# Six pieces of 128 to 512 tokens instead of 192 to 512, the weight split in quarters, and new orders of the engines' queues

## The reference

```python
# attention: q, k, v are (4, 8, 576, 64)
scores = scale * np.matmul(q, k.transpose(0, 1, 3, 2))
kth = np.partition(scores, -32, axis=-1)[..., -32:-31]
scores = np.where(scores >= kth, scores, -1e9)
attn = np.exp(scores - np.max(scores, axis=-1, keepdims=True))
attn = attn / (np.sum(attn, axis=-1, keepdims=True) + 1e-09)
x = attn @ v                      # laid out as (2304, 512)
# first MLP, d_ff 1536
x = (1 / (1 + np.exp(-(x @ w_gate))) * (x @ w_val)) @ w_out
# second MLP, d_ff 2048
r = np.maximum(x @ w_in, 0); out = (r * r) @ w_out2
```

## Time and profile before

| | |
|---|---|
| runs | 1176.04, 1176.14, 1177.05 us |
| profiled execution | 1176.16 us |
| its span | 1174.3 us |
| busy: PE, PEld | 1132.5 us (96%), 998.2 (85%) |
| busy: DVE, ACT, POOL | 838.3 (71%), 676.4 (58%), 623.5 (53%) |
| DMA | 270.13 MB, mean 230 GB/s |
| mean granted TensorE clock | 0.984 |

### The profile page before, as it was taken

One profiled execution on the slowest core, in us unless ns is written; L12 is line 12 of the kernel. 1 busy time (PEld: TensorE's weight loads), 2 busy tenths in 40 slices (PEclk: granted clock), 3 DMA queues, 4 the chain that ended last, 5 costly groups with the idle time before them and its releaser, 6 DMA issues.

```text
span 1174.3 us, 21809 instructions
## 1 busy us (share of the span) xinstructions
PE 1132.5 (96%) x7520; PEld 998.2 (85%) x7520; DVE 838.3 (71%) x1756; ACT 676.4 (58%) x1758; POOL 623.5 (53%) x539
## 2 busy tenths in 40 slices
PE   4579999999999999999999999999999999999999
PEld 2459989999989999999888787888888888899998
DVE  7999998788997898999777688975666683011130
ACT  5886777776875765776565557755544464112130
POOL 4987687776885555675445436643443365012130
PEclk7789999999999999999999999999999999999999
DMA  9988877988888666767655555665455555577784
GB/s 356 349 307 286 281 264 246 311 274 290 274 281 310 217 213 222 217 226 234 207 164 174 178 177 192 211 197 187 172 165 172 172 163 172 192 250 250 257 252 139
DMA packets 90397, 270.13 MB, mean 230 GB/s; under 512 B 10032, under 2 KB 16176, under 8 KB 90288
## 3 DMA queue, kind: packets, MB, share of 16 engines
q1 hardware_dynamic: 90288, 268.74, 68.5%
HBM read 228.33 MB, written 40.37 MB: 229 GB/s over the span
## 4 chain that ended last, share of the span: by engine, by line
PE 88%; DVE 7%; issue 2%; ACT 1%; SPq 1%; POOL 1%; DMA 1%; ACTq 0%; POOLq 0%
PE ps L648 21%; PE ps L650 21%; PE ps L649 21%; PE ps L634 7%; PE ps L589 7%; PE ps L549 6%; PE ps L565 5%; DVE work L850 3%; DVE top L848 3%; DMA heads_in<-qk_in 1%; SPq L470 1%; DVE g_lo L885 1%; POOL below L917 0%; POOL full_buf L957 0%; POOL probs L922 0%
## 5 line engine op out<-in xcount | busy, mean ns | idle before, releaser
L848 DVE MAX8 top<-work 128x8 f32<-128x576 f32 x432 | 312.3, 751 | 0.5
L917 POOL TENSOR_TENSOR below<-scores,below 128x576 f32<-128x576 f32 x120 | 174.2, 1451 | 237.8 <-ACT below L700 237.6
L648 PE MATMUL ps<-xy_hi,ring 128*128 128x512 f32 (+2 forms) x800 | 286.4, 358 | 0.0
L650 PE MATMUL ps<-xy_hi,ring 128*128 128x512 f32 (+2 forms) x800 | 281.4, 352 | 0.0
L649 PE MATMUL ps<-xy_lo,ring 128*128 128x512 f32 (+2 forms) x800 | 281.1, 351 | 0.0
L850 DVE MATCH_REPLACE8 work<-top,work 128x576 f32<-128x576 f32 x288 | 214.1, 743 | 0.0
L648 PE MATMUL ps<-g_hi,ring 128*128 128x384 f32 (+2 forms) x560 | 200.4, 358 | 0.3 <-DVE g_lo L885 0.3
L650 PE MATMUL ps<-g_hi,ring 128*128 128x384 f32 (+2 forms) x560 | 196.9, 352 | 0.0
L649 PE MATMUL ps<-g_lo,ring 128*128 128x384 f32 (+2 forms) x560 | 196.8, 351 | 0.0
L648 PEld LDWEIGHTS ps<-xy_hi,ring 128*128 128x128 f32 x800 | 150.2, 188 | 18.5 <-issue 6.9
L650 PEld LDWEIGHTS ps<-xy_hi,ring 128*128 128x128 f32 x800 | 150.1, 188 | 12.9
(11 more groups left out here) (70 smaller groups left out, 1709.8 us busy)
## 6 DMA issues: line engine op xcount, KB each, us to landing
ring<-w_split SPq DMA_DIRECT2D x318, 512.0 KB, 4.2
wring<-w_in SPq DMA_DIRECT2D x113, 256.0 KB, 5.3
w_split<-stage SPq DMA_DIRECT2D x46, 512.0 KB, 4.7
w_split<-ring SPq DMA_DIRECT2D x22, 512.0 KB, 6.0
vt<-v_in SPq DMA_DIRECT2D x16, 480.0 KB, 6.0
heads_in<-qk_in SPq DMA_DIRECT2D x16, 336.0 KB, 4.6
vt<-v_in SPq DMA_DIRECT2D x16, 320.0 KB, 3.2
heads_in<-qk_in SPq DMA_DIRECT2D x16, 304.0 KB, 4.4
```

The costliest lines, as they stand in the source:

```text
L648: nc.tensor.matmul(dst, w_hi, hi[:, k, 0:WIDTH[c]], start=first, stop=False)
L650: mm = nc.tensor.matmul(dst, w_lo, hi[:, k, 0:WIDTH[c]], start=False, stop=final)
L848: nc.vector.max(out=best, in_=sc if step == 0 else wk).then_inc(sel_step[t % 2], 1)
L917: nc.gpsimd.tensor_tensor(out=below[:, t % 2, :], in0=scores_of(t), in1=below[:, t % 2, :], op=ALU.subtract).then_inc(mask_done, 1)
```

## The change

The six pieces hold 128, 256, 384, 512, 512 and 512 tokens. WHEN sets which blocks are split when: of four, one ahead of the MLPs, one with the first piece and two beside the second. Margins in MLP_AT, the slot of turns in the later pieces (now t+3 everywhere but in the first), the slots of the splits ahead (0 to 9 now), and the order within a slot on ScalarE, VectorE and GpSimd change; it differs between the slots up to MLP_AT[2] and those from there on. TensorE's loop is written twice, with the old order in both. The planner's tables after: MLP_AT 11, 29, 55, 85, 118, 150; 18, 26, 30, 33 and 32 slots beside pieces one to five; 17 splits ahead, 17 with the first piece, 34 beside the second; 119 whole loads and 306 of both parts; 36 groups. Scores by stage 12+0, 4+0, 12+4, 11+7, 14+5, 11+0; turns 4+0, 9+0, 12+1, 12+7, 12+8, 15+0; products 4+0, 8+0, 13+1, 11+7, 12+8, 16+0.

```diff
--- before.py
+++ after.py
@@ -23,7 +23,7 @@
 KFULL = NBLK // 2
 
 
-PIECES = (((0, 0, 3),), ((1, 0, 5),), ((0, 3, 6),), ((1, 5, 4), (2, 0, 4)), ((2, 4, 5), (3, 0, 3)), ((3, 3, 6),))
+PIECES = (((0, 0, 2),), ((0, 2, 4),), ((1, 0, 6),), ((0, 6, 3), (2, 0, 5)), ((1, 6, 3), (3, 0, 5)), ((2, 5, 4), (3, 5, 4)))
 NC = len(PIECES)
 
 NW = 1
@@ -95,9 +95,10 @@
 AHEAD = 4
 STORE_LAG = 2
 CLASSES = NW + 2
-JOBS = [(None, n, True, True) for n in range(0, NB, CLASSES)]
+WHEN = [(0,1,2,2)[n % 4] for n in range(NB)]
+JOBS = [(None, n, True, True) for n in range(NB) if WHEN[n] == 0]
 NPRE = len(JOBS)
-JOBS += [(c, n, c + 1 == n % CLASSES, c < NW or c == NW and n % CLASSES == CLASSES - 1)
+JOBS += [(c, n, c + 1 == WHEN[n], c < NW or c == NW and WHEN[n] == CLASSES - 1)
          for c in range(NC) for n in range(NB)]
 NWHOLE = NPRE + NW * NB
 
@@ -144,14 +145,15 @@
 
 
 MASK = 2
-MLP_AT = [CHUNK_END[c] + (4, 6, 7, 7, 7, 7)[c] for c in range(NC)]
+MLP_AT = [CHUNK_END[c] + (4, 6, 8, 6, 7, 7)[c] for c in range(NC)]
 PAIRED = 2
+LATE = 1
 NORM_AT, TURN_AT, PROD_AT = {}, {}, {}
 for _t in range(NT):
-    _late = UNITS[TILES[_t][0]][0] > 0
+    _late = UNITS[TILES[_t][0]][0] >= LATE
     NORM_AT[_t + 2 + _late] = _t
     if _t in UNIT_AT:
-        TURN_AT[_t + 2 + _late + (UNITS[TILES[_t][0]][0] >= PAIRED)] = UNIT_AT[_t]
+        TURN_AT[_t + 2 + _late] = UNIT_AT[_t]
 TURN_SLOT = {u: s for s, u in TURN_AT.items()}
 
 
@@ -276,7 +278,7 @@
 
 SPLIT_AT = {}
 for _k in range(NPRE):
-    SPLIT_AT.setdefault(1 + _k * (MLP_AT[0] - 2) // NPRE, []).append(_k)
+    SPLIT_AT.setdefault(_k * (MLP_AT[0] - 1) // NPRE, []).append(_k)
 
 
 def attention_mlps(nc, qk, v, w, w_split, out):
@@ -656,7 +658,25 @@
-            for s in range(SLOTS):
+            for s in range(MLP_AT[2]):
...
+            for s in range(MLP_AT[2], SLOTS):
...
@@ -806,30 +826,54 @@
                 if s == MLP_AT[0] - 1:
                     for u in PROD_AT[s]:
                         copy_x(u)
-            for s in range(MLP_AT[0], SLOTS):
+            for s in range(MLP_AT[0], MLP_AT[2]):
+                if s - MASK < NT:
+                    find_below(s - MASK)
+                    enlarge(s - MASK)
+                for u in SCORE_AT.get(s - 1, [])[-1:]:
+                    for t in tiles_of(u):
+                        copy_scores(t)
+                for c, n in blocks_of(SHARES[s - 1][2]):
+                    evac(c, n)
+                if s - 1 in TURN_AT:
+                    copy_pt(TURN_AT[s - 1])
+                for c, p in X_AT.get(s, []):
+                    split_x(c, p)
+                for c, n in blocks_of(SHARES[s][0]):
+                    evac(c, n)
+                if s - MASK < NT:
+                    exp(s - MASK)
+                for u in SCORE_AT.get(s, [])[:-1]:
+                    for t in tiles_of(u):
+                        copy_scores(t)
+                for c, n in blocks_of(SHARES[s][1]):
+                    evac(c, n)
+                for u in PROD_AT.get(s, []):
+                    copy_x(u)
+            for s in range(MLP_AT[2], SLOTS):
                 for u in SCORE_AT.get(s - 1, [])[-1:]:
                     for t in tiles_of(u):
                         copy_scores(t)
                 if s - MASK < NT:
                     find_below(s - MASK)
                     enlarge(s - MASK)
-                for c, n in blocks_of(SHARES[s - 1][2]):
-                    evac(c, n)
                 if s - 1 in TURN_AT:
                     copy_pt(TURN_AT[s - 1])
+                for c, n in blocks_of(SHARES[s - 1][2]):
+                    evac(c, n)
                 for c, n in blocks_of(SHARES[s][0]):
                     evac(c, n)
                 for u in SCORE_AT.get(s, [])[:-1]:
                     for t in tiles_of(u):
                         copy_scores(t)
+                if s - MASK < NT:
+                    exp(s - MASK)
                 for c, p in X_AT.get(s, []):
                     split_x(c, p)
-                if s - MASK < NT:
-                    exp(s - MASK)
-                for c, n in blocks_of(SHARES[s][1]):
-                    evac(c, n)
                 for u in PROD_AT.get(s, []):
                     copy_x(u)
+                for c, n in blocks_of(SHARES[s][1]):
+                    evac(c, n)
             for c, n in blocks_of(SHARES[SLOTS - 1][2]) + blocks_of(REST):
                 evac(c, n)
 
@@ -850,12 +894,9 @@
                     nc.vector.match_replace(out=wk, in_to_replace=best, in_values=sc if step == 1 else wk,
                                             imm_value=-3.0e38).then_inc(sel_step[t % 2], 1)
 
-            def select_both(s, steps):
-                for step in steps:
-                    if 0 <= s - 1 < NT and step < 3:
-                        select(s - 1, 4 + step)
-                    if s < NT:
-                        select(s, step)
+            def select_if(t, step):
+                if 0 <= t < NT:
+                    select(t, step)
 
             def invert(t):
                 dve.wait_ge(sum_done, t + 1)
@@ -887,21 +928,42 @@
                                             op=ALU.subtract).then_inc(sq_lo_done, 1)
 
             dve.wait_ge(const_ready, 1)
-            for s in range(SLOTS):
-                if s in NORM_AT and s >= MLP_AT[0]:
+            for s in range(MLP_AT[2]):
+                if s in NORM_AT and UNITS[TILES[NORM_AT[s]][0]][0] >= LATE:
                     invert(NORM_AT[s])
+                select_if(s - 1, 4)
                 for c, n in blocks_of(SHARES[s - 1][2]) if s else []:
                     evac(c, n)
-                select_both(s, [0])
-                select_both(s, [1])
+                select_if(s, 0)
+                select_if(s - 1, 5)
                 for c, n in blocks_of(SHARES[s][0]):
                     evac(c, n)
-                select_both(s, [2])
-                if s in NORM_AT and s < MLP_AT[0]:
+                select_if(s, 1)
+                select_if(s - 1, 6)
+                select_if(s, 2)
+                for c, n in blocks_of(SHARES[s][1]):
+                    evac(c, n)
+                select_if(s, 3)
+                if s in NORM_AT and UNITS[TILES[NORM_AT[s]][0]][0] < LATE:
                     invert(NORM_AT[s])
+            for s in range(MLP_AT[2], SLOTS):
+                select_if(s, 0)
+                if s in NORM_AT and UNITS[TILES[NORM_AT[s]][0]][0] >= LATE:
+                    invert(NORM_AT[s])
+                select_if(s, 1)
+                for c, n in blocks_of(SHARES[s - 1][2]) if s else []:
+                    evac(c, n)
+                select_if(s - 1, 4)
+                select_if(s, 2)
+                if s in NORM_AT and UNITS[TILES[NORM_AT[s]][0]][0] < LATE:
+                    invert(NORM_AT[s])
+                select_if(s - 1, 5)
+                for c, n in blocks_of(SHARES[s][0]):
+                    evac(c, n)
                 for c, n in blocks_of(SHARES[s][1]):
                     evac(c, n)
-                select_both(s, [3])
+                select_if(s - 1, 6)
+                select_if(s, 3)
             for c, n in blocks_of(SHARES[SLOTS - 1][2]) + blocks_of(REST):
                 evac(c, n)
 
@@ -962,21 +1024,36 @@
             pool.wait_ge(const_step, 1)
             nc.gpsimd.affine_select(out=ident[:, :], in_=ident[:, :], compare_op=ALU.not_equal, fill=1.0,
                                     base=0, pattern=[[-1, P]], channel_multiplier=1).then_inc(const_ready, 1)
-            for s in range(SLOTS):
+            for s in range(MLP_AT[2]):
                 if 0 <= s - MASK < NT:
                     mask(s - MASK)
-                for c, n in blocks_of(SHARES[s - 1][2]) if s else []:
-                    evac(c, n)
-                for c, n in blocks_of(SHARES[s][0]):
-                    evac(c, n)
                 for k in SPLIT_AT.get(s - 1, []):
                     split_weights(k)
+                for c, n in blocks_of(SHARES[s - 1][2]) if s else []:
+                    evac(c, n)
                 if s in NORM_AT:
                     normalise(NORM_AT[s])
                 for c, p in X_AT.get(s, []):
                     split_x(c, p)
+                for c, n in blocks_of(SHARES[s][0]):
+                    evac(c, n)
                 for c, n in blocks_of(SHARES[s][1]):
                     evac(c, n)
+            for s in range(MLP_AT[2], SLOTS):
+                if 0 <= s - MASK < NT:
+                    mask(s - MASK)
+                for c, n in blocks_of(SHARES[s - 1][2]) if s else []:
+                    evac(c, n)
+                if s in NORM_AT:
+                    normalise(NORM_AT[s])
+                for c, n in blocks_of(SHARES[s][0]):
+                    evac(c, n)
+                for k in SPLIT_AT.get(s - 1, []):
+                    split_weights(k)
+                for c, n in blocks_of(SHARES[s][1]):
+                    evac(c, n)
+                for c, p in X_AT.get(s, []):
+                    split_x(c, p)
```

## The result

The changed kernel takes 1182.2 us in the median of 6 runs (1180.07 to 1184.03) against 1176.29 us for the kernel before (6 runs, 1176.01 to 1177.05): a ratio of 1.0049, interval 1.0035 to 1.0062. It is slower by half a per cent where I forecast half a per cent faster. The profiled execution took 1182.46 us, its span is 1180.6 us, and the mean granted clock of TensorE is 0.992 against 0.984.

The account below looks back on a forecast made before the run. VectorE was taken to bound the kernel up to slot 55 and TensorE from the third piece on: 308 + 859.9 = 1167.9 us of span, plus 1.9, gave 1170 us, 0.5% less. The range was 1157 to 1184.

Parts of the forecast that it names:

- Second piece ... Together 149.3: Slots 29 to 54: VectorE's selection 132.2 us, gate steps 5.6 and low parts 11.5, so slot 55 at 307.9.
- where VectorE is the slower one I take no lag: Third piece's start: TensorE begins with VectorE's slot 55, at 308 us, without the 1.9 us lag seen before.
- Start: Ahead of slot 11: late heads delay tile 3 by 3.7 us, to 24.0; first MLP matmul near 62 us.
- The first piece: Slots 11 to 28: VectorE paces with 91.5 us of selection and 2.4 of gate-times-value steps; slot 29 at 158.6.
- Prices: TensorE's MLP matmuls: 0.120 us at width 256 in fp32r, 0.109 per float32 record of 128 columns.
- the law: TensorE matmul time: columns at 2.4 GHz plus 0.013 us in fp32r, or plus 0.0025 us per float32 record.
- The low part at width 256: VectorE beside the second piece: 16 g_lo subtractions at 0.72 us each, bounds 0.40 to 1.5, together 11.5 us.
- rival D: Second piece: GpSimd at 90% makes low parts dearer, 0.95 us each, and splits delay turns: 1175; chance 0.09.
- From the third piece on: TensorE paces again and takes 859.9 us, against 803.7 in the kernel before.
- B: Later pieces: the reordered queues give back waits and changes between kinds, priced at 1160 us; chance 0.16.
- E: Later pieces: the earlier turn meets a late normalise, 0.1 us at 54 turns, 5 us: 1175; chance 0.09.
- C: Second piece: DMA paces it, 52 MB at 320 GB/s taking 162 us, 13 over VectorE's need: 1183; chance 0.24.

Follow-up runs that it names:

- e6: Changed kernel with six of seven selection steps of tiles 11 to 54 on 288 of 576 columns: 1177.32 us, ratio 1.0003.
- e2: Changed kernel without the 34 stores beside the second piece and the waits for them; output not the reference's: 1178.17 us, ratio 1.0014.
- e5: As e2, but with 34 stores of 480 KB from a spare buffer, for which no load waits: 1178.15 us, ratio 1.0007.
- e9: As e2, with GpSimd's normalise of tiles 26 to 51 covering only 64 of 576 columns: 1173.51 us, ratio 0.9977.
- e1: Changed kernel with blocks split in thirds again, 23 ahead, 23 with the first piece, 22 beside the second: 1197.33 us, ratio 1.0175.
- e13: Changed kernel, third group's heads after 8 weight blocks, stores one block earlier, splits 17, 23 and 28: 1180.41 us, ratio 1.0037.
- e14: As e13, but 20 blocks split ahead, 20 with the first piece, 28 beside the second: 1183.7 us, ratio 1.0062.
- e16: Changed kernel with the turns of the third piece one slot later (t + 4): 1179.89 us, ratio 1.0033.
- e15: As e16, plus third group's heads after 8 weight blocks and stores beside the second piece one block earlier: 1179.89 us, ratio 1.0022.
- e3: Changed kernel with the heads of the third group loaded after 8 weight blocks, not 16: 1179.44 us, ratio 1.0023.
- e8: Changed kernel with the kernel before's orders within a slot on ScalarE, VectorE and GpSimd: 1192.76 us, ratio 1.0121.

## Why the prediction was wrong

**The step that failed** is "Second piece ... Together 149.3", with "where VectorE is the slower one I take no lag". In VectorE's timeline the first MAX8 of tile 29 and that of tile 55 start at

```profile
159.76 0.74 DVE L892 MAX8 top<-scores 128x8 f32<-128x576 f32 x1
...
317.98 0.75 DVE L892 MAX8 top<-scores 128x8 f32<-128x576 f32 x1
```

That is 158.2 us, 8.9 more than the 149.3, and TensorE's third piece started 2.5 us behind slot 55. Slot 29 came 1.2 us late, and all else gave 0.2: together, but for rounding, the 12.7 us by which the span passes 1167.9. VectorE's work wasn't undersized: it was busy for 146.6 of the 158.2 us, 2.7 less than my sum. What I put at nothing, without a reason, is its idle time, 11.6 us. I had taken the busier engine for one that never waits. Nor was it clearly the busier one: TensorE, summed at 144 us, was busy for 150.8 in the piece. That VectorE paces the piece holds in the first (e6); in the second, VectorE, TensorE, GpSimd and DMA are all busy for 0.82 to 0.93 of the time and wait for each other in fixed orders.

Two causes are sized: the waits for stores in SyncE's queue 5.7 us (e2, e5), and 4.4 us that go when normalise is short (e9). With both gone the piece takes 151.8 us. These are single executions; the ratios of the totals give 0.35% for the one (1.0049 to 1.0014, 4.1 us) and 0.37% for the other (1.0014 to 0.9977, 4.4 us). Part of the first can be the clock: it stood at half for 10.2 us of the piece, and for 3.4 without the stores, which by my estimate is at most 3.4 us of TensorE's time. No run takes the two apart.

**What stays open** is the way in which the 4.4 us arise. Fewer splits don't bring them back (e1, e13, e14), nor does a later turn (e16 takes 1.6 us off, e15 adds 2.2). The chain from ScalarE's threshold over mask, exp and normalise to the turn runs through two queues twice; I haven't shown which place of it decides.

**Point by point.**
- Start. The mechanism was right, the size not: a stall of 5.1 us and tile 3 at 25.3 us instead of 24.0. The reciprocal of tile 0 came at 24.60 and not at 24.0, and behind it I had left out the MAX8 of tile 2 at 24.68 that stands ahead of tile 3, 0.66 us (e3 takes the stall away). The first MLP matmul is at 65.35 us, just outside 60 to 65.
- The first piece: 91.5 + 2.4 = 93.9 us from the slots. Slots 11 to 29 took 93.8, and TensorE's piece 93.3, paced by VectorE.
- Prices. At width 256, which the trace of before lacks, the law gave 0.120 us. Matmuls 2 and 24 of the second piece, in TensorE's timeline of the kernel after, are (161.46 - 158.83)/22 = 0.120 apart:

```profile
158.83 0.28 PE L651 MATMUL ps<-xy_lo,ring 128*128 128x256 f32 x1
...
161.46 0.28 PE L652 MATMUL ps<-xy_hi,ring 128*128 128x256 f32 x1
```

  A float32 record of 128 columns took 0.112 us (32 of them in 3.84 us and 20 in 2.50, from 65.35 us on) for 0.109.
- The low part at width 256, min/median/max in ns, of VectorE and of GpSimd:

```profile
L926 DVE TENSOR_TENSOR g_lo<-full_buf,g_hi x16: 406/602/1243, 246.9 to 287.1; 128x256 fp32r<-128x256 f32 x16
L1008 POOL TENSOR_TENSOR g_lo<-full_buf,g_hi x12: 727/742/754, 166.6 to 215.9; 128x256 fp32r<-128x256 f32 x12
```

  VectorE's mean is 0.75 us, close to the 0.72 that I took; rival D's price of 0.95 didn't come. One shape takes from 0.41 to 1.24 us on VectorE and always 0.73 to 0.75 on GpSimd. The Trainium skill ("SBUF — State Buffer", Who interferes with whom) has the two exclude each other for a whole instruction; the trace agrees. In 13 of the 16 a GpSimd instruction was running when VectorE's began, and each of the 13 ended 0.28 to 0.29 us after that one; the other three took 0.41 us. The mean that I worked out from the rule was too high.
- From the third piece on: 859.9 forecast, 860.1 measured. B is out, since the later pieces gave nothing back and the old orders give the same (e8). E is out for the later pieces: TensorE is busy there in all but some 3 us, at the end.
- C had the right sign and stretch, and part of the mechanism (whole loads that come late stop ScalarE and GpSimd). Its price was set in bytes, which e5 refutes for those of the stores; that its 1183 lies beside the measured 1182.2 is luck. I asked whether the rate sufficed, and not how long a load stands in the queue behind a wait. The earlier trace rows showed 2.6 us of such waits in slots of 6.7 us; SyncE's own waits, 38.2 us for stores in the second piece of before, I had left out.

The changed kernel also varies more, by 4.0 us between its six runs against 1.0: a stall that hangs on when a DMA lands may differ from one execution to the next, but only one of them was traced.

## What to carry to other kernels

When a stretch is made so short that several engines and DMA come over 0.8 of it, as here, treat the time of the busiest as a lower bound and not as the forecast; here 12.6 us came on top of 149.3, of which 5.7 hung on one in-order queue waiting for stores, and the stores' bytes cost nothing. Before such a change, list the waits of the queue that issues DMAs and ask what stands behind each. Then test with the waits taken away and the bytes kept: that tells a queue's order from its rate.

## What the runs showed of the hardware

- After the gap of 3.76 us on TensorE the granted clock stood at half from 217.0 to 220.4 us, and after one of 3.29 us again from 271.6 to 278.4. In e2, which has only the second of these gaps, 3.4 us at half are left in the second piece instead of 10.2; in the kernel before the clock stayed full from 75.8 us to the last 2 us. Matmuls of width 256 started 0.21 us apart at half and 0.12 at full, so a stall of a few us can cost TensorE more than its length.
- 34 stores of 480 KB among the loads took DMA from 222 to 321 GB/s and from a share of 0.69 to 0.91, and the piece's time didn't move (156.2 and 156.1 us).
- VectorE's subtraction with both inputs in SBUF (g_lo, 128x256) waits inside itself for the GpSimd instruction that is running, and then ends 0.28 us behind it: one that began at 268.88 us, with a split running on GpSimd until 269.84, took 1.24 us. GpSimd waits too: two splits that began inside such a subtraction took 1.46 and 1.50 us, the others 1.26 to 1.31; three normalises 1.33, the others 1.14 to 1.16. Both show up as longer instructions, not as idle time. In the kernel before, at width 320, 14 of the 16 subtractions of this kind in the second piece ended 0.34 to 0.35 us behind a GpSimd instruction.
